# Bonus product in the full array, flag product with 128 columns, and another order of the attention cluster on TensorE

## The chip, the cores and the metric

The kernel runs on one core of a Trainium2 chip. The metric is the device time of one execution in microseconds; lower is better. A measurement of this kernel can tell a difference of about 0.2% (0.67 us) from no change.

## What is computed

The reference chains three blocks. The change touches the first, a recurrence over 768 steps for 2 batches and 8 heads of 48 channels:

```
for t in range(S):
    cur = einsum('bhd,bhe->bhde', u * k[t], v[t])
    y[t] = einsum('bhd,bhde->bhe', r[t], state + cur)
    state = w[t][:, :, :, None] * state + einsum('bhd,bhe->bhde', k[t], v[t])
```

Its output `y`, as a matrix of 2 x 768 tokens by 384 channels, goes through a gated feed-forward block (token shift, then `k = relu(xk @ w_k)`, `v = k*k @ w_v`, `sigmoid(xr @ w_r) * v`), and then through a second one (`h = gelu(x @ w_in)`, half of it normalised and mixed along the sequence by `w_sg`, gate, `x + gated @ w_out`).

## The kernel before

The 1536 tokens are cut into 12 units of 128 steps; two units make one of six stages (`T = 256` tokens). For each unit the recurrence is done in chunk form with small float32 products on TensorE. A tile holds two heads, each on 64 of the 128 partitions (48 used), so eight heads are four pairs (`PAIRS = 4`), and a pair's product is written as two products, one for each half of the partitions. The products of a unit `un` are:

- `scores(un)`: decayed keys times decayed receptance, 64 rows and 128 columns of weights for each head, into `ps`. VectorE then masks them into `att` (`mask`, a predicated copy of 128x1024).
- `keys_by_step(un)`: four transposes of the keys into `pkt`; ScalarE copies them into `k_tok` (`keys`).
- `bonus(un)`: `u` times (r*k), summed over a head's channels and spread over its 64 rows: 64x64 weights taken from `par`, which ScalarE's DMA queue loads at the start. The moving operand `rkp` is GpSimd's product r*k. The result goes to `pm` for units 0 and 1 and to `pkt` after that.
- `from_state(un)`: the state before the chunk, read by the receptance, 64x64 weights, into `py`. It is left out for units 0 and 6, where a batch begins.
- `add_state(un)`: what the chunk adds to the state, 128x64 weights, into `pu`. VectorE takes it on in `carry_on`. Left out for units 5 and 11.
- `from_chunk(un)`: masked scores times the values, 128x64 weights, added in `py` to what `from_state` left.
- `flag_of(s)`: the sum over partitions of a check on the decays, one column of weights (`ones`), into row 0 of `pu` beside the state's columns. ScalarE adds it up, and SyncE and VectorE branch on it; with these inputs the branch isn't taken.

Every float32 product of this kind runs as two passes, so the trace has 16 MATMUL records for the eight products of `bonus`. The large products (lines 297 to 299, called MLP here) are in another float32 format, use the full array (128 x 128 weights) and run as three products of one pass each.

The order on TensorE is written out by hand. After a head with warm-up products (line 293), the stage loop puts the attention products of later units between groups of MLP products. One cluster of it is `outputs(un)`, most often followed by `scores(un + 1)`:

```
def outputs(un):
    bonus(un)
    from_state(un)
    add_state(un)
    from_chunk(un)
```

All other engines have such hand-written orders as well, and semaphores tie them. Unit 1 is an exception (`MOVED = 1`): its cluster stands in the head as `from_state(1)`, `bonus(1)`, `from_chunk(1)`, `move_last(1)`.

Of the kernel before, what the change touches and what calls it, by code (L numbers as in the profile page):

```python
# [10 lines left out]
ACT = mybir.ActivationFunctionType  # L11
AX = mybir.AxisListType

P = 128
C = 128
SLOT = 64
# [5 lines left out]
N = 2  # L22
# [11 lines left out]
def build(nc, r, k, v, w, u, units, vT, params, w_k, w_v, w_r, w_in, wsgT, b_sg, w_out, outT):  # L34
# [18 lines left out]
    with ctx:  # L53
# [12 lines left out]
        def put(name, at, dims, dt=F32):  # L66
            at += -at % 8
            t = nc.alloc_sbuf_tensor_at(name, [P, *dims], dt, offset=base + 4 * at)
            n = 1
            for d in dims:  # L70
                n *= d
            return t, at + n
# [87 lines left out]
        assert e <= r3  # L160

        x2, e = put("x2", r3, [KT, B * S])
        par, e = put("par", e, [PAIRS * SLOT + 2 * KT + GT])
        u_b = par[:, 0:PAIRS * SLOT].rearrange("p (g e) -> p g e", g=PAIRS)
        mu = par[:, PAIRS * SLOT:PAIRS * SLOT + 2 * KT].rearrange("p (n t) -> p n t", n=2)
        gln = par[:, PAIRS * SLOT + 2 * KT:]
        omu, e = put("omu", e, [2, KT])
        outside, e = put("outside", e, [NU])
        flags, e = put("flags", e, [NU])
        flag, e = put("flag", e, [STAGES])  # L170
        ones, e = put("ones", e, [1])
        minus_one, e = put("minus_one", e, [1])
        half_neg, e = put("half_neg", e, [1])
        stats, e = put("stats", e, [ST, 6])
# [16 lines left out]
        def bonus_bank(un):  # L191

            return pm[un] if un < 2 else pkt
# [406 lines left out]
        def _(pe):  # L600
# [26 lines left out]
            def bonus(un):  # L627

                pe.wait_ge(s_par, 16)
                pe.wait_ge(rkp_done, un + 1)  # L630
                if un >= 2:
                    pe.wait_ge(ktok_done, states(un + 1))
                    pe.wait_ge(bonus_done, un)
                for g in range(PAIRS):
                    cols = slice(g * C, (g + 1) * C)
                    for h in range(2):
                        head = slice(h * SLOT, (h + 1) * SLOT)
                        mm = pe.matmul(bonus_bank(un)[head, cols], u_b[head, g], rkp[head, un % 2, cols],  # L638
                                       start=True, stop=True)
                mm.then_inc(c_mm, 1)  # L640

            def flag_of(s):

                pe.wait_ge(checked, N * (s + 1))
                pe.wait_ge(state_done, states(N * s + 1))
                pe.matmul(pu[0:1, STATE:STATE + N * (s + 1)], ones[:], outside[:, 0:N * (s + 1)],
                          start=True, stop=True).then_inc(flag_mm, 1)

            def add_state(un):
# [15 lines left out]
            def from_state(un):  # L665

                if place(un)[2] == 0:
                    return
                pe.wait_ge(state_done, states(un))
                if un >= 2:  # L670
                    pe.wait_ge(y_done, un)
                    pe.wait_ge(main_done, un)
                for g in range(PAIRS):
                    cols = slice(g * C, (g + 1) * C)
                    for h in range(2):
                        head = slice(h * SLOT, (h + 1) * SLOT)
                        pe.matmul(y_bank(un)[head, cols], state[head, (un - 1) % 2, g], r_in[head, un % 2, cols],  # L677
                                  start=g == 0, stop=False, skip_group_check=True)

            def from_chunk(un):  # L680

                first = place(un)[2] == 0
                pe.wait_ge(s_v[un % 3], 16 * (un // 3 + 1))
                pe.wait_ge(att_done, un + 1)
                if first and un >= 2:
                    pe.wait_ge(y_done, un)
                    pe.wait_ge(main_done, un)
                for g in range(PAIRS):
                    cols = slice(g * C, (g + 1) * C)
                    for h in range(2):  # L690
                        mm = pe.matmul(y_bank(un)[h * SLOT:(h + 1) * SLOT, cols], vb[:, un % 3, g, h, :],  # L691
                                       att[:, un % 2, h, cols], start=first and g == 0, stop=g == PAIRS - 1,
                                       skip_group_check=True)
                mm.then_inc(y_mm, 1)

            def move_last(un):

# [39 lines left out]

            def outputs(un):
                bonus(un)
                from_state(un)  # L740
                add_state(un)
                from_chunk(un)

            warm(pe, 4)
            scores(0)
# [105 lines left out]
        def _(act):  # L851
            act.dma_start(par[:], params).then_inc(s_par, 16)
            act.wait_ge(s_const, 7)
            act.activation(tables[:, 0:1], ones[:], ACT.Sigmoid).then_inc(s_sig, 1)

            def by_head(t):
                return t.rearrange("p (h e) -> p h e", h=2)
# [109 lines left out]
            for s in range(STAGES):  # L967
                a, b = 2 * s + 2, 2 * s + 3
                if s == 0:
                    gate(s, *RS[0])  # L970
                    high_weight(wv[0])
                    gate(s, *RS[1])
                    keys(1)
                    high_weight(wv[1])
                    key_high(s, 0)
                    check(a)
                    keys(a)
                    key_high(s, 1)
                    high_weight(wv[2])
                    check(b)  # L980
                    keys(b)
                    flag_out(s + 1)
                    key_high(s, 2)
                    high_weight(wv[3])
                    key_high(s, 3)
                    mix(s + 1)
                    keys(b + 1)
                elif s < STAGES - 1:
                    gate(s, *RS[0])
                    check(a)  # L990
                    check(b)
                    gate(s, *RS[1])
                    keys(b)
                    key_high(s, 0)
                    flag_out(s + 1)
                    for n in range(1, KG):
                        key_high(s, n)
                    mix(s + 1)
                    if b + 1 < NU:
                        keys(b + 1)  # L1000
                else:
                    gate(s, *RS[0])
                    gate(s, *RS[1])
                    act.activation(tables[:, 1:2], ones[:], ACT.Gelu_apprx_tanh).then_inc(s_sig, 1)
                    key_high(s, 0)
                    for n in range(1, KG):
                        high_weight(parts_of("win")[n - 1])
                        key_high(s, n)
                    split_x2(0)
# [331 lines left out]
def lay_out(inputs):  # L1341
# [5 lines left out]
    for un in range(B * S // C):  # L1347
# [13 lines left out]
                v_un[:, g, h, 0:D] = v[b, 2 * g + h, t]  # L1361
        units += [w_un, rkv_un.reshape(P, 3 * WIDE)]
        vT.append(v_un.reshape(C, WIDE))
    u_b = _np.zeros((P, PAIRS, SLOT), _np.float32)
    for g in range(PAIRS):
        for h in range(2):
            u_b[h * SLOT:h * SLOT + D, g] = u[2 * g + h][:, None]
    order = []
    for j in range(PAIRS - 1):
        for h in range(2):  # L1370
# [4 lines left out]
    arrays = {n: inputs[n] for n in "rkvwu"}  # L1375
    arrays["units"] = _np.concatenate(units, axis=1)
    arrays["vT"] = _np.concatenate(vT, axis=1)
    arrays["params"] = _np.concatenate([u_b.reshape(P, PAIRS * SLOT), *by_row], axis=1)
    arrays["moe_w_k"] = inputs["moe_w_k"][order]
    arrays["moe_w_v"] = inputs["moe_w_v"]  # L1380
    arrays["moe_w_r"] = inputs["moe_w_r"][order]
# [20 lines left out]
```

## Time and profile before

| | us |
|---|---|
| median of 3 runs (lowest, highest) | 333.68 (333.19, 333.71) |
| the profiled execution's own time | 332.61 |
| its span in the profile | 330.9 |
| TensorE matmul busy | 320.0 (97%) |
| TensorE weight load busy | 299.5 (91%) |
| VectorE busy | 197.2 (60%) |
| ScalarE busy | 151.0 (46%) |
| GpSimd busy | 98.1 (30%) |

The granted TensorE clock is full in all 40 slices of the page. Busy time of TensorE's matmuls counts overlapping records once. A matmul's record is longer than the distance to the next one (an MLP product's is 0.28 us long, and the next starts 0.12 us later), so costs on TensorE are read as distances between starts.

### The profile page before, as it was taken

What the parts mean: (1) busy time and instruction counts of PE and PEld (TensorE: products, weight loads), DVE (VectorE), ACT (ScalarE), POOL (GpSimd) and SP (SyncE); (2) the same over time, 40 slices, a digit from 0 to 9 for tenths busy, and PEclk for the clock granted to TensorE, in tenths of its full rate; (3) what the DMA queues carried; (4) which work ended last, traced back from release to release, by engine and by line L of the source; (5) the groups of instructions that cost most, each with busy time, mean ns of one, the idle gap of its engine ahead of it and who ended that gap; (6) DMA issues with size and microseconds to landing.
All of it is one profiled execution on the core that took longest, in us unless ns stands there. A gap on an engine that the chain in (4) does not pass through costs nothing.

```text
span 330.9 us, 6786 instructions
## 1 busy us (share of the span) xinstructions
PE 320.0 (97%) x2684; PEld 299.5 (91%) x2684; DVE 197.2 (60%) x331; ACT 151.0 (46%) x301; POOL 98.1 (30%) x94
## 2 busy tenths in 40 slices
PE   6987899999999999999999999999999999999996
PEld 2657889999999999999999998899999988999996
DVE  4869999983696398639416055991643546123432
ACT  5446844553845455465547592755113025311100
POOL 5530344004314211430032050672233018313220
PEclk9999999999999999999999999999999999999999
DMA  7979033232304401300006036000000210000012
GB/s 230 408 259 350 27 124 125 87 130 61 144 2 165 166 5 24 144 9 2 6 9 240 0 110 246 29 0 0 2 0 0 97 49 0 2 0 2 0 48 95
DMA packets 11153, 28.09 MB, mean 85 GB/s; under 512 B 1232, under 2 KB 5872, under 8 KB 9840
## 3 DMA queue, kind: packets, MB, share of 16 engines
q1 hardware_dynamic: 10976, 27.51, 23.7%
q8 instruction: 21, 0.34, 0.4%
q10 hardware_dynamic: 144, 0.14, 0.1%
q14 instruction: 12, 0.10, 0.1%
HBM read 24.74 MB, written 2.36 MB: 82 GB/s over the span
## 4 chain that ended last, share of the span: by engine, by line
PE 84%; DVE 7%; ACT 3%; issue 2%; DMA 2%; POOL 0%; SPq 0%; ACTq 0%; DVEq 0%
PE pm L297 16%; PE pm L298 15%; PE pm L299 15%; PE ps L613 3%; PE ps L297 3%; PE ps L299 3%; PE ps L298 3%; PE py L691 3%; PE pkt L638 3%; PE py L677 2%; PE pkt L297 2%; PE pkt L299 2%; PE pu L297 2%; PE pu L299 2%; PE pkt L298 2%
## 5 line engine op out<-in xcount | busy, mean ns | idle before, releaser
L542 POOL TENSOR_TENSOR k_l<-sq,k_h 128x512 fp32r<-128x512 f32 x24 | 31.9, 1332 | 79.2 <-ACT sq L944 79.2
L297 PE MATMUL pm<-xkr_h,wk_h 128*128 128x256 f32 x144 | 42.1, 292 | 0.0
L297 PE MATMUL pm<-k_h,wv_h 128*128 128x256 f32 x144 | 41.2, 286 | 0.4 <-POOL k_l L542 0.4
L299 PE MATMUL pm<-k_h,wv_l 128*128 128x256 f32 x144 | 40.7, 283 | 0.0
L298 PE MATMUL pm<-k_l,wv_h 128*128 128x256 f32 x144 | 40.7, 283 | 0.0
L298 PE MATMUL pm<-xkr_l,wk_h 128*128 128x256 f32 x144 | 40.7, 283 | 0.0
L299 PE MATMUL pm<-xkr_h,wk_l 128*128 128x256 f32 x144 | 40.7, 282 | 0.0
L533 POOL TENSOR_TENSOR rkp<-inw 128x512 f32<-128x512 f32 x12 | 15.3, 1281 | 62.7 <-DVE r_in L1132 62.7
L936 ACT ACTIVATE relu<-pm 128x512 f32<-128x512 f32 x24 | 14.3, 596 | 36.2 <-PE pm L299 36.1
L595 POOL TENSOR_TENSOR gated_l<-gf,gated_h 128x384 fp32r<-128x384 f32 x16 | 16.4, 1025 | 46.1 <-ACT gated_h L1055 36.1
L1187 DVE SCALAR_TENSOR_TENSOR xf<-X,omu,xf 128x256 f32<-128x256 f32 x36 | 19.5, 554 | 15.4 <-ACT xf L902 15.4
L297 PEld LDWEIGHTS pm<-xkr_h,wk_h 128*128 128x128 f32 x144 | 27.5, 191 | 1.0 <-issue 0.3
L297 PEld LDWEIGHTS pm<-k_h,wv_h 128*128 128x128 f32 x144 | 27.6, 192 | 0.7 <-issue 0.6
L1055 ACT CAST gated_h<-gf 128x384 fp32r<-128x384 f32 x16 | 8.2, 514 | 42.9 <-DVE gf L1330 42.9
L298 PEld LDWEIGHTS pm<-k_l,wv_h 128*128 128x128 f32 x144 | 27.6, 192 | 0.0
L299 PEld LDWEIGHTS pm<-k_h,wv_l 128*128 128x128 f32 x144 | 27.6, 192 | 0.0
L298 PEld LDWEIGHTS pm<-xkr_l,wk_h 128*128 128x128 f32 x144 | 27.6, 191 | 0.0
L299 PEld LDWEIGHTS pm<-xkr_h,wk_l 128*128 128x128 f32 x144 | 27.5, 191 | 0.0
L902 ACT ACTIVATE xf<-X,par 128x256 f32<-128x256 f32 x36 | 17.6, 503 | 5.9 <-DMA X<-y 5.9
L1139 DVE COPY_PREDICATED att<-upper,ps 128x1024 f32<-128x1024 uint32 x12 | 16.3, 1360 | 3.5 <-PE ps L613 3.4
L569 POOL TENSOR_TENSOR rstd<-vare,half_neg 128x1 f32<-128x1 f32 x12 | 9.3, 779 | 29.4 <-DVE vare L1308 29.4
L577 POOL TENSOR_TENSOR vn_l<-vf,vn_h 128x512 fp32r<-128x512 f32 x12 | 17.2, 1436 | 2.2 <-ACT vn_h L1016 2.2
(239 smaller groups left out, 880.4 us busy)
## 6 DMA issues: line engine op xcount, KB each, us to landing
inw<-in_units SPq DMA_DIRECT2D x10, 1026.5 KB, 5.0
vb<-in_vT SPq DMA_DIRECT2D x12, 256.0 KB, 5.0
wsg_raw<-in_wsgT SPq DMA_DIRECT2D x1, 2304.0 KB, 8.8
out_y<-y_out SPq DMA_DIRECT2D x12, 192.0 KB, 1.9
wk_raw<-in_moe_w_k SPq DMA_DIRECT2D x3, 512.0 KB, 9.9
wv_raw<-in_moe_w_v SPq DMA_DIRECT2D x4, 384.0 KB, 7.0
win_raw<-in_moe_w_in SPq DMA_DIRECT2D x3, 512.0 KB, 4.6
inw<-in_units SPq DMA_DIRECT2D x2, 512.0 KB, 5.5
```

Of the source, the lines that this page charges most:

```text
L297: pe.matmul(o, a_h, b_h, start=first and n == 0, stop=False, skip_group_check=True)
L298: pe.matmul(o, a_h, b_l, start=False, stop=False, skip_group_check=True)
L299: mm = pe.matmul(o, a_l, b_h, start=False, stop=last and n == len(pairs) - 1, skip_group_check=True)
L533: pool.tensor_tensor(rkp[:, un % 2], inw[:, un % 3, W1:W1 + WIDE], inw[:, un % 3, W1 + WIDE:W1 + 2 * WIDE], ALU.mult).then_inc(rkp_done, 1)
L542: pool.tensor_tensor(k2_l[:, 2 * n:2 * n + 2], sq[:, j % 2].rearrange("p (g t) -> p g t", g=2), k2_h[:, 2 * n:2 * n + 2], ALU.subtract).th ...
L577: pool.tensor_tensor(vn_l[:, t], vf[:, n % 2], vn_h[:, t], ALU.subtract).then_inc(vnl_done, 1)
L595: pool.tensor_tensor(gated_l[:, x, cols], gf[:, ng % 2], gated_h[:, x, cols], ALU.subtract).then_inc(gl_done, 1)
L613: mm = pe.matmul(ps[:, h, cols], k_in[head, p, cols], r_in[head, p, cols], start=True, stop=True)
L902: act.activation(xf[:, kt, n], X[:, s % 2, kt, 1:T + 1], ACT.Identity, scale=mu[:, n, kt:kt + 1]).then_inc(t_done, 1)
L936: act.activation(relu[:, j % 2], pm[bk][:], ACT.Relu).then_inc(m_free[bk], 1)
L1139: dve.copy_predicated(att[:, un % 2].rearrange("p h (g t) -> p h g t", g=PAIRS), upper[:].bitcast(U32).unsqueeze(1).unsqueeze(1).to_broadc ...
L1187: dve.scalar_tensor_tensor(out=xf[:, kt, n], in0=X[:, s % 2, kt, 0:T], scalar=omu[:, n, kt:kt + 1], in1=xf[:, kt, n], op0=ALU.mult, op1=AL ...
```

## The change

The weights of `bonus` become block-diagonal: `u_b` has 128 columns for each pair, with a head's `u` in its own 64x64 block and zeros elsewhere. One product in the full array then does both heads, so `bonus` issues four products where it issued eight. `par` grows from 266 to 522 columns, and so does the DMA that loads it. `flag_of` uses `ones` with 128 columns (a 128x128 memset on GpSimd where it was 128x1) and writes the sum into all 128 rows. In `outputs` the state reads move behind the chunk's product; so `from_chunk` now opens the accumulation in `py` and does the waiting for that bank, and `from_state` closes it and signals `y_mm`. For unit 1 the roles stay as they were.

```
-        par, e = put("par", e, [PAIRS * SLOT + 2 * KT + GT])
-        u_b = par[:, 0:PAIRS * SLOT].rearrange("p (g e) -> p g e", g=PAIRS)
+        par, e = put("par", e, [PAIRS * P + 2 * KT + GT])
+        u_b = par[:, 0:PAIRS * P].rearrange("p (g e) -> p g e", g=PAIRS)
...
-        ones, e = put("ones", e, [1])
+        ones, e = put("ones", e, [P])
...
                 for g in range(PAIRS):
                     cols = slice(g * C, (g + 1) * C)
-                    for h in range(2):
-                        head = slice(h * SLOT, (h + 1) * SLOT)
-                        mm = pe.matmul(bonus_bank(un)[head, cols], u_b[head, g], rkp[head, un % 2, cols],
-                                       start=True, stop=True)
+                    mm = pe.matmul(bonus_bank(un)[:, cols], u_b[:, g], rkp[:, un % 2, cols], start=True, stop=True)
                 mm.then_inc(c_mm, 1)
...
-                pe.matmul(pu[0:1, STATE:STATE + N * (s + 1)], ones[:], outside[:, 0:N * (s + 1)],
+                pe.matmul(pu[:, STATE:STATE + N * (s + 1)], ones[:], outside[:, 0:N * (s + 1)],
                           start=True, stop=True).then_inc(flag_mm, 1)
...
                 pe.wait_ge(state_done, states(un))
-                if un >= 2:
-                    pe.wait_ge(y_done, un)
-                    pe.wait_ge(main_done, un)
                 for g in range(PAIRS):
...
-                        pe.matmul(y_bank(un)[head, cols], state[head, (un - 1) % 2, g], r_in[head, un % 2, cols],
-                                  start=g == 0, stop=False, skip_group_check=True)
+                        mm = pe.matmul(y_bank(un)[head, cols], state[head, (un - 1) % 2, g], r_in[head, un % 2, cols],
+                                       start=un == MOVED and g == 0, stop=un != MOVED and g == PAIRS - 1,
+                                       skip_group_check=True)
+                if un != MOVED:
+                    mm.then_inc(y_mm, 1)
...
             def from_chunk(un):
 
-                first = place(un)[2] == 0
                 pe.wait_ge(s_v[un % 3], 16 * (un // 3 + 1))
                 pe.wait_ge(att_done, un + 1)
-                if first and un >= 2:
+                if un >= 2:
                     pe.wait_ge(y_done, un)
                     pe.wait_ge(main_done, un)
+                alone = place(un)[2] == 0 or un == MOVED
...
             def outputs(un):
                 bonus(un)
-                from_state(un)
                 add_state(un)
                 from_chunk(un)
+                from_state(un)
...
-    u_b = _np.zeros((P, PAIRS, SLOT), _np.float32)
+    u_b = _np.zeros((P, PAIRS, P), _np.float32)
     for g in range(PAIRS):
         for h in range(2):
-            u_b[h * SLOT:h * SLOT + D, g] = u[2 * g + h][:, None]
+            u_b[h * SLOT:h * SLOT + D, g, h * SLOT:(h + 1) * SLOT] = u[2 * g + h][:, None]
```

The order of TensorE's instructions at unit 2 in stage 0, behind the second group of key products of the MLP (`rkp,par` is `bonus`, `r_in,state` is `from_state`, `vb,k_tok` is `add_state`, `att,vb` is `from_chunk`; the shape is that of the output, x8 the number of products):

```order
-L638 MATMUL pkt<-rkp,par 64x128 x8
-L677 MATMUL py<-r_in,state 64x128 x8
-L661 MATMUL pu<-vb,k_tok 64x64 x8
-L691 MATMUL py<-att,vb 64x128 x8
+L636 MATMUL pkt<-rkp,par 128x128 x4
+L658 MATMUL pu<-vb,k_tok 64x64 x8
+L688 MATMUL py<-att,vb 64x128 x8
+L671 MATMUL py<-r_in,state 64x128 x8
 L613 MATMUL ps<-r_in,k_in 128x128 x8
 L624 MATMUL pkt<-ident,k_in 128x128 x4
```

The eight state reads stand last in the cluster now, behind the chunk's product and in front of the next unit's scores.

The head of TensorE's order, before, from the scores of unit 1 on (`outside,ones` is `flag_of`):

```order
L613 MATMUL ps<-r_in,k_in 128x128 x8
L638 MATMUL pm<-rkp,par 64x128 x8
L646 MATMUL pu<-outside,ones 1x2
L691 MATMUL pm<-att,vb 64x128 x8
L677 MATMUL py<-r_in,state 64x128 x8
L638 MATMUL pm<-rkp,par 64x128 x8
L691 MATMUL py<-att,vb 64x128 x8
```

And the same place of the change:

```order
L613 MATMUL ps<-r_in,k_in 128x128 x8
L636 MATMUL pm<-rkp,par 128x128 x4
L643 MATMUL pu<-outside,ones 128x2
L688 MATMUL pm<-att,vb 64x128 x8
L671 MATMUL py<-r_in,state 64x128 x8
L636 MATMUL pm<-rkp,par 128x128 x4
L688 MATMUL py<-att,vb 64x128 x8
```

Here nothing has moved; the two bonus products and the flag have changed their shapes. The orders of the other engines are the same but for the sizes of `par` and `ones`.

## Rows read from the trace of the kernel before

**Rows 1.** The page's busy times, share of the span and instructions
```profile
PE 320.0 (97%) x2684; PEld 299.5 (91%) x2684; DVE 197.2 (60%) x331; ACT 151.0 (46%) x301; POOL 98.1 (30%) x94
```

**Rows 2.** Stretches: length, busy of PE, PEld, DVE, ACT, POOL; clock, DMA, GB/s
```profile
42.00:202.00 160.00, 159.62 (x1669) 152.87 (x1666) 105.79 (x177) 88.93 (x186) 41.05 (x32) 1.00 0.26 89
202.00:331.00 129.00, 125.93 (x697) 121.36 (x695) 58.34 (x103) 37.06 (x66) 41.97 (x40) 1.00 0.08 25
```

**Rows 3.** Waits of TensorE from 42 us to the end: total us, times, longest
```profile
PE pm L297 <- POOL k_l L542: 0.4, 1, 0.4
```

**Rows 4.** Timeline of TensorE around the cluster of unit 3: start us, length us
```profile
46.16 0.28 PE L299 MATMUL pm<-xkr_h,wk_l 128*128 128x256 f32 x1
46.37 1.09 PE L638 MATMUL pkt<-rkp,par 64*64 64x128 f32 x16
47.30 1.04 PE L677 MATMUL py<-r_in,state 64*64 64x128 f32 x16
48.27 0.69 PE L661 MATMUL pu<-vb,k_tok 128*64 128x64 f32 x16
48.78 1.04 PE L691 MATMUL py<-att,vb 128*64 128x128 f32 x16
49.76 0.39 PE L297 MATMUL pm<-xkr_h,wk_h 128*128 128x256 f32 x1
49.98 0.28 PE L298 MATMUL pm<-xkr_l,wk_h 128*128 128x256 f32 x1
```

**Rows 5.** The same timeline around the cluster of unit 2
```profile
37.97 1.09 PE L638 MATMUL pkt<-rkp,par 64*64 64x128 f32 x16 [0.18 <-issue]
...
39.86 0.69 PE L661 MATMUL pu<-vb,k_tok 128*64 128x64 f32 x16
41.20 1.10 PE L691 MATMUL py<-att,vb 128*64 128x128 f32 x16 [0.65 <-DVE att L1139]
42.22 1.16 PE L613 MATMUL ps<-r_in,k_in 64*128 64x128 f32 x16
```

**Rows 6.** Timeline of VectorE: the mask of unit 2
```profile
39.69 1.36 DVE L1139 COPY_PREDICATED att<-upper,ps 128x1024 f32<-128x1024 uint32 x1
```

**Rows 7.** Timeline of weight loads: six float32 passes in the full array
```profile
20.44 0.74 PEld L701 LDWEIGHTS py<-y,moves 128*128 128x128 f32 x6 [0.70 <-issue]
21.11 0.30 PEld L293 LDWEIGHTS pm<-one,ident 128*128 128x128 f32 x2
```

**Rows 8.** Timeline of TensorE around the flag of stage 2
```profile
72.30 0.28 PE L299 MATMUL pm<-xkr_h,wk_l 128*128 128x256 f32 x1
72.51 0.19 PE L646 MATMUL pu<-outside,ones 128*1 128x6 f32 x2
...
72.86 0.28 PE L298 MATMUL pm<-xkr_l,wk_h 128*128 128x256 f32 x1
```

**Rows 9.** Timeline of TensorE in the head
```profile
15.97 1.09 PE L691 MATMUL pm<-att,vb 128*64 128x128 f32 x16
17.00 1.09 PE L677 MATMUL py<-r_in,state 64*64 64x128 f32 x16
```

**Rows 10.** DMA queues from 1.8 to 4.4 us, and the page's row on par
```profile
q1 hardware_dynamic: 222, 0.58, 75.0%
q10 hardware_dynamic: 144, 0.14, 16.4%
...
par<-in_params ACTq DMA_DIRECT2D x1, 133.0 KB, 3.5
```

**Rows 11.** Timelines of VectorE and ScalarE in the head
```profile
0.79 0.41 ACTq L852 DMA_DIRECT2D par<-in_params  x1
...
4.26 1.23 DVE L1110 TENSOR_TENSOR_SCAN prod<-inw,one 128x516 f32<-128x516 f32 x1 [4.26 <-DMA inw<-in_units]
...
21.41 0.56 DVE L1176 TENSOR_TENSOR X<-py,inw 128x384 f32<-128x384 f32 x1
...
22.24 0.91 ACT L902 ACTIVATE xf<-X,par 128x256 f32<-128x256 f32 x2 [4.14 <-DMA X<-y]
```

More of the change, by code:

```diff
@@ L162, in build @@
         x2, e = put("x2", r3, [KT, B * S])
-        par, e = put("par", e, [PAIRS * SLOT + 2 * KT + GT])
-        u_b = par[:, 0:PAIRS * SLOT].rearrange("p (g e) -> p g e", g=PAIRS)
-        mu = par[:, PAIRS * SLOT:PAIRS * SLOT + 2 * KT].rearrange("p (n t) -> p n t", n=2)
-        gln = par[:, PAIRS * SLOT + 2 * KT:]
+        par, e = put("par", e, [PAIRS * P + 2 * KT + GT])
+        u_b = par[:, 0:PAIRS * P].rearrange("p (g e) -> p g e", g=PAIRS)
+        mu = par[:, PAIRS * P:PAIRS * P + 2 * KT].rearrange("p (n t) -> p n t", n=2)
+        gln = par[:, PAIRS * P + 2 * KT:]
         omu, e = put("omu", e, [2, KT])
@@ L691, in from_chunk @@
                         mm = pe.matmul(y_bank(un)[h * SLOT:(h + 1) * SLOT, cols], vb[:, un % 3, g, h, :],
-                                       att[:, un % 2, h, cols], start=first and g == 0, stop=g == PAIRS - 1,
-                                       skip_group_check=True)
-                mm.then_inc(y_mm, 1)
+                                       att[:, un % 2, h, cols], start=un != MOVED and g == 0,
+                                       stop=alone and g == PAIRS - 1, skip_group_check=True)
+                if alone:
+                    mm.then_inc(y_mm, 1)
             def move_last(un):
@@ L853, in _ @@
             act.wait_ge(s_const, 7)
-            act.activation(tables[:, 0:1], ones[:], ACT.Sigmoid).then_inc(s_sig, 1)
+            act.activation(tables[:, 0:1], ones[:, 0:1], ACT.Sigmoid).then_inc(s_sig, 1)
             def by_head(t):
@@ L1003, in _ @@
                     gate(s, *RS[1])
-                    act.activation(tables[:, 1:2], ones[:], ACT.Gelu_apprx_tanh).then_inc(s_sig, 1)
+                    act.activation(tables[:, 1:2], ones[:, 0:1], ACT.Gelu_apprx_tanh).then_inc(s_sig, 1)
                     key_high(s, 0)
@@ L1377, in lay_out @@
     arrays["vT"] = _np.concatenate(vT, axis=1)
-    arrays["params"] = _np.concatenate([u_b.reshape(P, PAIRS * SLOT), *by_row], axis=1)
+    arrays["params"] = _np.concatenate([u_b.reshape(P, PAIRS * P), *by_row], axis=1)
     arrays["moe_w_k"] = inputs["moe_w_k"][order]
```

## Prediction

> **What bounds the kernel now.** I read the page's busy times first. TensorE is busy for 97% of the span, and no other engine for more than 60% [rows 1]. Such a share is an average, so I looked at stretches next. From 42 to 202 us TensorE is busy 159.62 us of 160, and from 202 us on 125.93 of 129, of which the last piece is the tail of the output [rows 2]. The view of waits confirms it: from 42 us to the end TensorE waits once, for 0.4 us [rows 3]. The reader should see that from 42 us on TensorE's own time is the kernel's time. Each 0.1 us added to its instructions there, or taken from them, arrives at the end.
>
> Before 42 us it is otherwise. The first work starts when a DMA has landed, at 4.26 us on VectorE [rows 11], and unit 2's `from_chunk` waits 0.65 us for the mask `att`, which VectorE finishes at 39.69 + 1.36 = 41.05 us [rows 5, 6]. So TensorE is tied to VectorE once more at 41.05 us, and only what moves that point, or comes behind it, counts.
>
> **The change part by part.** The sum is made against the profiled execution's own 332.61 us. The median of the runs, 333.68, lies 1.07 above it; I add the change to the median.
>
> *What a change of array shape costs.* The records name the part of the array: 64*64, 128*64, 128*128. Where it changes, the pairs of starts are further apart. `from_chunk` of unit 3 takes 48.78 to 49.76 = 0.98 with a change behind it and none ahead; that of unit 0 takes 15.97 to 17.00 = 1.03 with one on both sides [rows 4, 9]. So coming in costs 0.05. `bonus` of unit 3 takes 0.93 with a change ahead and none behind, so sixteen passes take 0.88, and going out costs 0.10. MLP products follow each other by 0.12; going out of them takes 0.21 (46.16 to 46.37), and coming back 0.22 (49.76 to 49.98), so 0.09 and 0.10 more [rows 4].
>
> *Bonus in the full array.* Eight passes in place of sixteen, which looks like half. But the sixteen run two by two: 0.88 us for eight pairs is 0.11 for a pair. A full-array float32 pass with 128 moving columns has a row too, the products with `moves`: six passes from 20.44 to 21.11, 0.112 each [rows 7]. Eight take 0.89. The two halves already ran side by side, so nothing is gained in the product itself.
>
> The Trainium skill ("TensorE: Matmul & The Clock Gate", Back-to-back issue gap) gives about 81 ns for a product with 128 moving columns in a sustained stream. By it the eight passes would take 0.65 us, and the sum would be about 2.2 us lower over the nine clusters behind unit 2's. The trace disagrees, with 0.112 us for a pass of this very kind.
>
> *The cluster of unit 3.* Before: 0.21 + 0.93 + 0.97 + 0.51 + 0.98 + 0.22 = 3.82 [rows 4]. After: MLP to bonus has no change of shape, 0.12. Bonus with a change behind it, 0.89 + 0.10 = 0.99. `add_state`, 0.51, as before with a change ahead. `from_chunk` 0.98. `from_state`, now with a change on both sides, 0.05 + 0.88 + 0.10 = 1.03. MLP 0.22. Sum 3.85, so 0.03 more. The change of shape that the bonus no longer needs ahead of it comes back between the chunk's product and the state reads: three changes before, three after. With scores behind the cluster both have one more. Eight clusters are like this one (units 3, 4, 5 and 7 to 11; without `add_state` the difference is the same), +0.24. Unit 6 has no state reads, so there the saved change isn't given back: 0.09 + 0.05 + 0.88 + 0.10 - 0.99 = 0.13 less. Together +0.11. No row shows a change from 64*64 to 128*128 or 64*128; if it cost nothing, the eight would save 0.10 each more (-0.8), and if it cost as much again, +0.8. All other kinds in the rows agree within 0.01 us, so I take 0.10.
>
> *The flag.* It takes 72.30 to 72.86 = 0.56 where two steps of 0.12 would be 0.24, so 0.32 for a product of a few columns: two changes of shape [rows 8]. In the full array it needs none, and is two passes of at most 0.112: 0.22. Five flags stand behind 42 us: 5 x (0.32 - 0.22) = -0.50. Bounds: -0.3 (some of it stays) to -1.0 (passes with so few columns cost 0.02).
>
> *The cluster of unit 2.* This is where the new order costs. Before, TensorE ran the state reads while the mask was being made, and then waited 0.65 us. Now they stand behind `from_chunk`, which can't start before `att` (41.05 us) however early TensorE gets there. Bonus and additions end by 37.97 + 0.99 + 0.51 = 39.5, and the wait grows from 0.65 to about 1.7 us. From 41.20 on the chunk's product takes 1.02 as before [rows 5], and then 1.03 of state reads come before the scores that stood at 42.22. Queued behind them are the scores of unit 3, the mask of unit 3 and all MLP products. Nothing hides this: TensorE has no wait behind 42 us that could shrink but the one of 0.4, which comes from a chain that is moved with it. So +1.03, between 0.9 and 1.1. At no other unit does the mask bind: unit 3's chunk starts without a wait at 48.78 [rows 4], and moves up by one block only.
>
> *The larger par.* It has 256 more columns, 131 KB. Its 144 packets run between 1.8 and 4.4 us beside those that VectorE's first scan waits for, with 91% of the 16 engines' time taken; its own share is 16.4% of 2.6 us, 0.43 us [rows 10]. It is nearly doubled, so the scan's data land up to 0.42 us later if all of the new bytes are served ahead of them, and 0 if none. Both land within 0.2 us of each other (0.79 + 3.5 = 4.3 for par, 4.26 for the scan's start [rows 10, 11]), so they are served side by side. I take +0.35. From the scan the chain runs through VectorE without a pause, so this moves 41.05 and all that follows.
>
> The Trainium skill ("DMA: Bandwidth & Descriptors", the queue model) says that each DMA engine goes round the queues that have work, packet by packet. By that rule most of par's new bytes come ahead of the scan's last ones, which is the upper end; the trace, with both landing together, agrees.
>
> *The rest of the head.* Bonus 0, the flag and unit 0's chunk stay within 0.05: 0.89 + 0.22 against 1.02 + 0.12. Unit 1's bonus gets changes ahead and behind, some 0.15 later; its `X` is written at 21.41 + 0.56 = 21.97, with 0.27 to spare to 22.24 [rows 11]. I take +0.05 for both. The wider memset of `ones` (0.1 us or so) is over long before 4.26 us.
>
> Sum: 0.11 - 0.50 + 1.03 + 0.35 + 0.05 = +1.04. That gives 333.65 for a profiled execution, and 333.68 + 1.04 = 334.7 for the median, 0.3% slower.
>
> **The rivals.**
> 1. *The head hides par.* The extra bytes fall into gaps of the DMA engines (9% are free). Then the sum is +0.7: 334.4. For it: the share isn't 100%. Against it: the two transfers land together. Chance 0.15.
> 2. *The stall of unit 2 isn't new time*, because the mask comes earlier than in the old trace or TensorE arrives there later anyway. Then the sum is about 0: 333.7. Against it: VectorE is at work without a pause up to the mask, and its order is unchanged. Chance 0.08.
> 3. *Faster: a change in one direction only (rows or columns) costs less than one in both.* In the new order each change inside a cluster is in one direction. If both changes that the state reads now have were free, eight clusters would save 0.3 each, -2.4: 332.3. It decides from 0.22 us per cluster on, where the sum falls under -0.67. Against it: 64*64 to 128*64 (rows only) costs 0.10 in unit 3, and 128*64 to 128*128 (columns only) 0.10 as well, no less than the others [rows 4]. Chance 0.05.
> 4. *Faster: a full-array pass is paced by its moving columns.* An MLP product has 256 and takes 0.12 [rows 4]; half of that is 0.06, eight passes 0.48, and nine clusters would save 0.41 each: -3.7, 331.0. Against it: the six passes at 0.112 [rows 7]. Chance 0.02. (The Trainium skill's 81 ns, in the section named above, would stand between the two.)
> 5. *Slower still: a change that no row shows (64*64 straight to 128*128 or 64*128) is dearer.* With 0.1 us more in each of nine clusters, 335.6. Chance 0.1.
>
> The forecast keeps 0.6, with 334.2 to 335.2 as its own range.
>
> **How the numbers follow.** A measurement can tell about 0.2%, 0.67 us: 333.0 to 334.35 is no change. Slower holds the forecast but for a sliver (0.57), half of rival 1 and all of rival 5: 0.74. Same: that sliver, half of rival 1 and rival 2: 0.19. Faster: rivals 3 and 4, 0.07. The range leaves out rivals 3 and 4, most of 5 and some of 2: 333.7 to 335.4.
>
> **What would show it.** In the new profile: `from_chunk` of unit 2 waits about 1.7 us for `att`; its scores start 1.0 us later than the mask's shift alone explains; bonus blocks take 0.99 from start to start and follow MLP by 0.12; the cluster of unit 3 takes 3.85; a flag takes 0.22 over its neighbours; the first scan starts near 4.6 us. The prediction is wrong if the scan starts at 4.26 as before, if unit 2's wait stays under 1 us, or if the cluster of unit 3 is shorter than 3.7.

## The result and the profile after

The changed kernel takes 334.07 us (median of 22 runs, 333.72 to 334.43), the kernel before 333.33 (22 runs, 332.44 to 333.90). The ratio is 1.0022 with a 95% interval of 1.0015 to 1.0029: slower by 0.74 us, inside the predicted range of 333.7 to 335.4 and on the predicted side, less than the 1.04 us of the sum. It isn't a clear hit: 334.07 lies under the forecast's own range (334.2 to 335.2) and, counted from the older median 333.68, inside the band 333.0 to 334.35 that the prediction calls no change, to which it gave 0.19. The median of before over 22 runs is 0.35 lower than that of the first three. The profiled execution took 333.90, 1.29 above that of before.

The page of the changed kernel: the span, the busy times, and ScalarE's DMA queue, which carries `par`:

```profile
span 332.2 us, 6594 instructions
...
PE 320.1 (96%) x2588; PEld 300.8 (91%) x2588; DVE 198.7 (60%) x331; ACT 151.0 (45%) x301; POOL 97.8 (29%) x94
...
q10 hardware_dynamic: 144, 0.27, 0.2%
```

TensorE has 96 records fewer (48 products of two passes) and is busy as long as before [rows 1]: half as many bonus passes take the same time. The queue carries 0.13 MB more.

The timeline of TensorE at unit 2, where [rows 5] are the rows of before:

```profile
38.72 1.13 PE L636 MATMUL pkt<-rkp,par 128*128 128x128 f32 x8 [0.27 <-issue]
39.78 0.69 PE L658 MATMUL pu<-vb,k_tok 128*64 128x64 f32 x16
41.82 1.09 PE L688 MATMUL py<-att,vb 128*64 128x128 f32 x16 [1.35 <-issue]
42.84 1.09 PE L671 MATMUL py<-r_in,state 64*64 64x128 f32 x16
43.87 1.16 PE L613 MATMUL ps<-r_in,k_in 64*128 64x128 f32 x16
```

VectorE's mask for that unit:

```profile
40.37 1.35 DVE L1137 COPY_PREDICATED att<-upper,ps 128x1024 f32<-128x1024 uint32 x1
```

The chunk's product now idles 1.35 us and starts 0.10 after the mask's end at 41.72. The prediction's 1.7 is counted between starts; counted so it is 1.52 (39.78 + 0.52 to 41.82). The profile puts that wait down to "issue", but the mask is what ends just ahead of it, as in [rows 5, 6]. The mask starts 0.68 later than in [rows 6]; unit 3's scores start 1.65 later than in [rows 5] (43.87 for 42.22). So 0.97 us are new at this place.

The cluster of unit 3, to be held against [rows 4]:

```profile
47.71 0.28 PE L299 MATMUL pm<-xkr_h,wk_l 128*128 128x256 f32 x1
47.83 1.05 PE L636 MATMUL pkt<-rkp,par 128*128 128x128 f32 x8
48.81 0.69 PE L658 MATMUL pu<-vb,k_tok 128*64 128x64 f32 x16
49.33 1.04 PE L688 MATMUL py<-att,vb 128*64 128x128 f32 x16
50.30 1.09 PE L671 MATMUL py<-r_in,state 64*64 64x128 f32 x16
51.32 0.39 PE L297 MATMUL pm<-xkr_h,wk_h 128*128 128x256 f32 x1
51.55 0.28 PE L298 MATMUL pm<-xkr_l,wk_h 128*128 128x256 f32 x1
```

From start to start: 0.12 into the bonus, 0.98 for it, 0.52, 0.97, 1.02, 0.23: 3.84 us in all, against 3.82 before.

The flag of stage 2, for [rows 8]:

```profile
73.90 0.28 PE L299 MATMUL pm<-xkr_h,wk_l 128*128 128x256 f32 x1
74.02 0.28 PE L643 MATMUL pu<-outside,ones 128*128 128x6 f32 x2
...
74.36 0.28 PE L298 MATMUL pm<-xkr_l,wk_h 128*128 128x256 f32 x1
```

0.46 us where it was 0.56. And the head, for [rows 11]: VectorE's first scan and the two rows on which ScalarE's first product with `mu` hangs:

```profile
4.76 1.23 DVE L1108 TENSOR_TENSOR_SCAN prod<-inw,one 128x516 f32<-128x516 f32 x1 [4.76 <-DMA inw<-in_units]
...
22.19 0.56 DVE L1174 TENSOR_TENSOR X<-py,inw 128x384 f32<-128x384 f32 x1
...
22.92 0.91 ACT L900 ACTIVATE xf<-X,par 128x256 f32<-128x256 f32 x2 [4.46 <-DVE X L1174]
```

The scan starts 0.50 later. ScalarE's product starts 0.68 later and is released by `X` of unit 1, no longer by the DMA as in [rows 11]. `X` itself is 0.78 late (22.19 for 21.41), 0.28 of it behind the scan. That comes from TensorE, at unit 1's bonus and chunk, before:

```profile
17.92 1.04 PE L638 MATMUL pm<-rkp,par 64*64 64x128 f32 x16
18.89 1.09 PE L691 MATMUL py<-att,vb 128*64 128x128 f32 x16
```

and now:

```profile
18.58 1.16 PE L636 MATMUL pm<-rkp,par 128*128 128x128 f32 x8
19.67 1.09 PE L688 MATMUL py<-att,vb 128*64 128x128 f32 x16
```

The full-array bonus takes 1.09 from start to start for 0.97, and the state reads ahead of it 1.02 for 0.92 (17.56 to 18.58, before 17.00 to 17.92). Unit 0's bonus, flag and chunk add 0.07 (0.99 + 0.22 for 1.02 + 0.12). Of these 0.28 us 0.10 are hidden: the product starts 0.17 after the end of `X` (22.19 + 0.56 = 22.75, 22.92), so before, `X` had 0.10 to spare and not 0.27.

The whole way of these 1.3 us in the two traces: +0.50 at the first scan, +0.18 in the rest of the head, +0.97 at unit 2, and -0.35 from unit 3's scores to the end (332.2 - 43.87 = 288.33 for 330.9 - 42.22 = 288.68). The medians differ by 0.74 only. The experiments are about that gap as much as about the terms.

### The profile page after: what moved, and what is told of

It is laid out like the page before. It is cut to its first block, busy times and chain, and to the rows that moved or that the text cites. A ratio compares the mean times of both kernels' runs of the same rounds, so it can differ in the third digit from the quotient of the medians.

```text
span 332.2 us, 6594 instructions
## 1 busy us (share of the span) xinstructions
PE 320.1 (96%) x2588; PEld 300.8 (91%) x2588; DVE 198.7 (60%) x331; ACT 151.0 (45%) x301; POOL 97.8 (29%) x94
## 4 chain that ended last, share of the span: by engine, by line
PE 88%; DVE 5%; ACT 3%; issue 2%; DMA 1%; POOL 0%; ACTq 0%; DVEq 0%
PE pm L297 16%; PE pm L298 16%; PE pm L299 16%; PE ps L613 4%; PE ps L297 3%; PE ps L298 3%; PE ps L299 3%; PE py L688 3%; PE py L671 3%; PE pkt L636 3%; PE pu L658 2%; PE pkt L297 2%; PE pkt L298 2%; PE pkt L299 2%; PE pu L297 2%
```

## The experiments

Each kernel was timed in 6 or 12 runs beside the kernel before on the same chip. Every run also lists the mean clock granted over the span, which turned out to matter. For reading them together, this table has five figures of each profile (us): the start of the first scan, the start of the mask of unit 2, the start of the scores of unit 3, the span, and the rest from those scores to the end of the span, in which TensorE alone sets the time.

| kernel | first scan | mask of unit 2 | scores of unit 3 | span | rest | median of runs |
|---|---|---|---|---|---|---|
| before | 4.26 | 39.69 | 42.22 | 330.9 | 288.68 | 333.33 |
| changed | 4.76 | 40.37 | 43.87 | 332.2 | 288.33 | 334.07 |
| par wide only | 4.74 | 40.05 | 43.20 | 331.9 | 288.70 | 333.64 |
| order only | 4.06 | 39.64 | 43.15 | 333.1 | 289.95 | 334.98 |
| unit 2 in old order | 4.68 | 40.28 | 43.60 | 331.9 | 288.30 | 333.84 |
| all in old order | 4.99 | 40.57 | 43.08 | 331.4 | 288.32 | 333.67 |
| before, 4 products filled in | 4.15 | 39.50 | 42.39 | 331.1 | 288.71 | 333.25 |
| changed, 4 filled in | 4.61 | 40.23 | 43.72 | 332.0 | 288.28 | 334.00 |
| flag wide, 4 filled in | 4.30 | 40.38 | 43.27 | 331.5 | 288.23 | 332.73 |
| unit 2 old, 4 filled in | 4.83 | 40.47 | 43.55 | 331.9 | 288.35 | 333.61 |
| before, 2 filled in | 4.29 | 39.61 | 42.13 | 330.8 | 288.67 | 332.76 |
| changed, 2 filled in | 4.70 | 40.30 | 43.79 | 332.1 | 288.31 | 333.99 |
| unit 2 old, 2 filled in | 4.84 | 40.45 | 42.97 | 331.3 | 288.33 | 332.96 |
| flag wide, par late, 2 filled in | 3.75 | 40.59 | 43.12 | 331.3 | 288.18 | 332.59 |

**Par alone.** The kernel before with `par` padded by zeros to the new width:

```
-    arrays["params"] = _np.concatenate([u_b.reshape(P, PAIRS * SLOT), *by_row], axis=1)
+    arrays["params"] = _np.concatenate([u_b.reshape(P, PAIRS * SLOT), _np.zeros((P, PAIRS * SLOT), _np.float32), *by_row], axis=1)
```

> The kernel before, with par widened from 266 to 522 columns by zeros that nothing reads; all else as before. If par's new bytes come ahead of the data of the first scan, the scan starts near 4.7 us in the profile where it was 4.26, and the time rises by 0.4 to 0.5 us. If they fall into free time of the DMA engines, both stay and the time is that of before within 0.2 us.

Measured: the scan starts at 4.74 for 4.26, so the DMA term is real, and somewhat above its upper bound of 0.42. One pair of profiles would not carry that, but all of them do: the scan starts at 4.06 to 4.30 in the five with the small par loaded first (4.21 on the average), and at 4.61 to 4.99 in the eight with the large one (4.77). The time is 333.64 against 333.35 of the kernel before beside it, ratio 1.0011 (0.9998 to 1.0024): some 0.3 us, which the interval doesn't tell from none. The trace held something unlooked for. A stretch of this profile (length, busy of PE, PEld, DVE, ACT and POOL with counts, granted clock, DMA share, GB/s):

```profile
31.00:34.00 3.00, 2.71 (x24) 2.59 (x25) 2.93 (x5) 0.97 (x2) 0.25 (x1) 0.59 0.85 340
```

In the profile of before it reads:

```profile
31.00:34.00 3.00, 3.00 (x36) 2.80 (x37) 2.93 (x5) 0.61 (x2) 0.61 (x1) 1.00 0.65 230
```

and its timeline has these rows of TensorE behind the wait for `k_tok`:

```profile
30.93 0.69 PE L661 MATMUL pu<-vb,k_tok 128*64 128x64 f32 x16 [2.12 <-ACT k_tok L888]
...
33.89 1.16 PE L613 MATMUL ps<-r_in,k_in 64*128 64x128 f32 x16
```

The timeline of TensorE with par wide, behind the transposes of unit 1 and then at unit 2:

```profile
31.29 0.95 PE L661 MATMUL pu<-vb,k_tok 128*64 128x64 f32 x16 [2.13 <-ACT k_tok L888]
...
32.55 0.41 PE L298 MATMUL pm<-xkr_l,wk_h 128*128 128x256 f32 x1
32.77 0.41 PE L299 MATMUL pm<-xkr_h,wk_l 128*128 128x256 f32 x1
...
35.73 1.16 PE L613 MATMUL ps<-r_in,k_in 64*128 64x128 f32 x16
...
42.22 1.05 PE L691 MATMUL py<-att,vb 128*64 128x128 f32 x16
43.20 1.16 PE L613 MATMUL ps<-r_in,k_in 64*128 64x128 f32 x16
```

TensorE waits 2.13 us for `k_tok`. When it goes on, its clock is at half, the lower of its two levels, 1.2 GHz: products of 0.41 us that follow each other by 0.21 where they were 0.28 and 0.12. The scores behind that group of key products start at 35.73 for 33.89: 1.84 us later, 0.36 of which were there at the end of the wait (31.29 for 30.93), so the drop costs 1.5. At unit 2 TensorE therefore comes later than the mask (41.40) and doesn't wait for it: the chunk's product starts 0.82 behind the mask's end, where 0.15 is usual, so 0.67 of the 1.5 us get through. In the profile of before the same wait of 2.12 us was not followed by a drop. So two kinds of executions exist, and the mean clock tells them apart: in the profiles it is 0.995 where the drop occurred (three) and 0.999 or 1.000 where not; that it is the same drop in the executions that were only timed is inferred from this. Of the 99 timed executions of the kernel before whose clock is listed (29, 35 and 35, on three chips), 71 had a mean of 0.994 or 0.995 and took 333.54 (median), 28 had 0.999 or 1.000 and took 332.51. (The expectation below that speaks of 18 of 26 miscounts: it was 21 of 29.) Of the changed kernel 11 had it (334.15) and 11 not (333.99).

By kinds, par alone costs 0.86 us where there was no drop (7 runs, 333.31; before 8 runs, 332.45) and 0.17 with it (333.79 for 333.62). Also, the 1.0 us between the two kinds of the kernel before is more than the 0.67 that the trace shows of the drop. The kinds differ in the head as well: in the three profiles with the drop unit 0's scores start without a wait behind TensorE's warm-up products, in the three without it and without the filling described below they wait 0.20 to 0.60 us for VectorE. What ties the two together is not shown.

So TensorE's lateness and its wait at unit 2 are alternatives. Where the clock has dropped, the time that the new order loses at unit 2 had been lost before TensorE got there.

**Order alone.** The new order with the 64x64 bonus, the flag of one column and the small par:

```
-                    mm = pe.matmul(bonus_bank(un)[:, cols], u_b[:, g], rkp[:, un % 2, cols], start=True, stop=True)
+                    for h in range(2):
+                        head = slice(h * SLOT, (h + 1) * SLOT)
+                        mm = pe.matmul(bonus_bank(un)[head, cols], u_b[head, g], rkp[head, un % 2, cols],
+                                       start=True, stop=True)
```

> The new order of the cluster with the old products (bonus 64x64, flag with one column, small par). If changes of array shape are what counts, each cluster now has four of them where it had three: unit 3 takes 3.82 + 0.15 = 3.97 us, eight clusters add 1.2 us, unit 2 adds 1.0 for its wait, in all about +2.2 us. If the order costs only by the wait of unit 2, +1.0 us. If shapes that differ in one direction only changed cheaply, less than +1.0.

Measured: 334.98 (6 runs), ratio 1.0064 (1.0045 to 1.0083), so 1.6 us over before where 2.2 was expected. The cluster of unit 3:

```profile
47.28 1.09 PE L638 MATMUL pkt<-rkp,par 64*64 64x128 f32 x16
48.30 0.69 PE L661 MATMUL pu<-vb,k_tok 128*64 128x64 f32 x16
...
49.79 1.09 PE L674 MATMUL py<-r_in,state 64*64 64x128 f32 x16
50.81 0.39 PE L297 MATMUL pm<-xkr_h,wk_h 128*128 128x256 f32 x1
```

The bonus takes 1.02 and the state reads 1.02, where 0.93 and 0.97 stand in [rows 4]: each is now shut in between two changes of shape. The rest behind unit 3's scores is 1.27 us longer than before; 1.2 was expected for eight clusters. The order by itself saves nothing. It adds a change of shape to each cluster, and the wide bonus takes one away. Unit 2's loss hardly shows, since five of the six runs had the drop: their median is 335.01, 1.39 over the 21 runs of before beside them that had it too (333.62), little more than those 1.27.

**Unit 2 alone in the old order.**

```
+        STATE_FIRST = (MOVED, 2)
...
             def outputs(un):
                 bonus(un)
+                if un in STATE_FIRST:
+                    from_state(un)
                 add_state(un)
                 from_chunk(un)
-                from_state(un)
+                if un not in STATE_FIRST:
+                    from_state(un)
```

(with the start and stop flags, the wait for the bank and the signal moved accordingly)

> The changed kernel, but in unit 2's cluster alone the state reads stand ahead of the additions and the chunk's product again. If the longer wait of unit 2 for its mask is new time, this is 1.0 us faster than the changed kernel (333.1 where that is 334.07). If the wait is made good later, both are the same.

Measured: 333.84, 0.2 under the changed kernel and not 1.0. A miss, if one looks at medians. By the clock it is a hit, if on few runs: the 4 runs without the drop have a median of 332.96, the changed kernel's 11 such runs 333.99, so 1.03 us; the 8 with the drop 333.95, against 334.15, so 0.20.

**All clusters in the old order**, with the wide products (`STATE_FIRST = tuple(range(NU))`).

> The changed kernel's wide bonus, flag and par with the old order in all clusters. By the count of changes of shape, three for the cluster of unit 3 in this order too, it takes 3.85 us as in the changed kernel, and the time equals that of the kernel whose unit 2 alone has the old order, within 0.2 us (1.0 us under the changed kernel). If the order is worth something by itself (changes in one direction only are cheaper), it is slower than that one by 0.1 us or more per cluster, 0.8 us in all.

Measured: 333.67, ratio to before 1.0019 (1.0006 to 1.0032), 0.17 from the kernel with unit 2 alone in the old order, with 332.99 and 333.89 by the clock. The rest is 288.32 for 288.30 there and 288.33 in the changed kernel. Which way round the products stand doesn't matter behind unit 2; what counts is the number of changes of shape, and it is the same. The rival of cheap changes in one direction is out.

**Filling the wait.** If idleness precedes the drop, work in its place should keep the clock up, and show the change at its full price. Four warm-up products went into the wait for `k_tok` at unit 1, in four kernels:

```
                     keys_by_step(1)
+                    warm(pe, 4)
                     add_state(1)
```

> The kernel before, with four warm-up products (line 293, 1.7 us at full clock, results not used) in the 2.1 us in which TensorE waits for k_tok at unit 1. In 18 of 26 timed executions of the kernel before the mean clock was 0.995, and in the profiles with that mean the granted clock was at 0.5 from about 31.4 to 34.8 us; those executions took 1.0 us longer. If what precedes the drop is the idle stretch, no execution has it now, and all are near 332.5. If the drop has nothing to do with it, two in three still have it and the median stays near 333.4.

Measured: 333.25, ratio to before 1.0005 (0.9993 to 1.0017). All 12 runs have a mean clock of 1.000 or 0.999, so the drop is gone, yet the time isn't near 332.5. The timeline shows my error:

```profile
28.43 3.60 PE L293 MATMUL pm<-one,ident 128*128 128x512 f32 x8
31.96 0.69 PE L661 MATMUL pu<-vb,k_tok 128*64 128x64 f32 x16
```

Four products are eight passes, 3.5 us, not the 1.7 that the expectation says. They overfill the wait: the additions start 1.0 us later (31.96 for 30.93), and [rows 5] show that TensorE had 0.8 left at unit 2 (39.86 + 0.52 to 41.20). That explains some 0.2 to 0.4 us. The profiled execution, 332.77, was the fastest of the twelve; what the others took on top, up to 333.76, no trace shows, but the head, which differs between executions as told below, could be the place.

> The changed kernel with the same four products in the same wait. At full clock it took 333.99, with the drop 334.15, as TensorE has 1.4 us to spare ahead of unit 2's mask. If the drop is gone, 334.0, and the distance to the kernel before with the same filling is the full price of the change, 1.5 us, twice what was measured without the filling. The rival, that the change costs 0.7 us whatever the clock does, gives 0.7 us over it.

Measured: 334.00, ratio 1.0026 (1.0015 to 1.0038). The time is as expected; the distance to the filled kernel before is 0.75 and not 1.5, since that one was itself late.

> The changed kernel with unit 2 in the old order and with the filling. If the state reads behind unit 2's mask cost 1.0 us at full clock and less only where the clock had dropped, this is 1.0 us faster than the changed kernel with the filling (333.0). Without filling the difference of the medians was 0.2 us.

Measured: 333.61, 0.39 under the changed kernel with the same filling, again because TensorE comes late by the filling.

The fourth, the kernel before with the wide flag alone:

```
-                pe.matmul(pu[0:1, STATE:STATE + N * (s + 1)], ones[:], outside[:, 0:N * (s + 1)],
+                pe.matmul(pu[:, STATE:STATE + N * (s + 1)], ones[:], outside[:, 0:N * (s + 1)],
```

> The kernel before with the filling, and the flag product alone widened to 128 columns. By the prediction's term the five flags behind 42 us save 0.5 us against the filled kernel before (332.0 where that is 332.5). If the passes are paced by their weight loads more slowly than the rows of before suggest, or nothing of a change of shape is saved, 0.0 to 0.2.

Measured: 332.73, 0.52 under the filled kernel before; the rest is 288.23 for 288.71. This doesn't hang on unit 2, so the term of the flag stands. In this kernel the wide flag costs something in the head: between unit 0's bonus (64*64) and chunk (128*64) it takes 0.32 (16.43 to 16.75) where the narrow one took 0.12.

**Filling it with two products** (1.7 us) gives the test that the four had spoilt.

> The kernel before with two warm-up products in the wait for k_tok where the earlier filling had four: four took 3.5 us (line 293 runs as two passes of 0.43 us), 1.1 us more than the wait, and so cost what they were to save. Two take 1.7 us and fit. If the drop of the clock follows the idle stretch, it is gone here too, and the median is 332.5, as in the executions of the kernel before without a drop, 0.9 under its median. If 0.6 us of idleness is enough, the drop stays in part and the median is near 333.3.

Measured: 332.76 (332.41 to 333.84), 0.53 under before by the medians; the ratio is 0.9993, and its interval, 0.9981 to 1.0006, doesn't exclude that nothing was gained. No run has the drop. The wait is filled but for 0.41 us, and TensorE waits for the mask of unit 2 again:

```profile
31.00:34.00 3.00, 3.00 (x36) 2.80 (x36) 2.93 (x5) 0.61 (x2) 0.69 (x1) 1.00 0.92 343
```

```profile
28.55 1.88 PE L293 MATMUL pm<-one,ident 128*128 128x512 f32 x4
30.85 0.69 PE L661 MATMUL pu<-vb,k_tok 128*64 128x64 f32 x16 [0.41 <-ACT k_tok L889]
...
41.11 1.09 PE L691 MATMUL py<-att,vb 128*64 128x128 f32 x16 [0.55 <-DVE att L1140]
42.13 1.16 PE L613 MATMUL ps<-r_in,k_in 64*128 64x128 f32 x16
```

> The changed kernel with two products in the wait. TensorE waits for unit 2's mask at either clock, so the filling gives nothing: 334.0, 1.5 us over the filled kernel before. If the change costs 0.7 us whatever the clock does, it is 0.7 over that.

Measured: 333.99, ratio to before 1.0027 (1.0015 to 1.0039), and 1.23 us above the filled kernel before. The filling gives the changed kernel nothing, and before 0.5. That is the price of the change with the clock held up, well over the 0.74 of the plain medians. It is not quite the 1.5 expected, which is also the distance between the runs without a drop when nothing is filled (333.99 for 332.51, 1.48); the two profiles with filling are 1.3 apart in span, as are the two without. So the price is 1.2 to 1.5, and the sum's 1.04 lies under all of these.

> The changed kernel with unit 2 in the old order and two products in the wait. By the price of the state reads at full clock 1.0 us under the changed kernel with the same filling, 333.0. If the reads behind the mask cost only what the medians without filling showed, 0.2 us under it.

Measured: 332.96 (332.79 to 333.30), 1.03 under the changed kernel with the same filling. At unit 2 the changed kernel with two products has these rows,

```profile
41.75 1.09 PE L688 MATMUL py<-att,vb 128*64 128x128 f32 x16 [1.33 <-issue]
...
43.79 1.16 PE L613 MATMUL ps<-r_in,k_in 64*128 64x128 f32 x16
```

and with unit 2 in the old order these:

```profile
39.78 1.09 PE L675 MATMUL py<-r_in,state 64*64 64x128 f32 x16
...
41.94 1.09 PE L692 MATMUL py<-att,vb 128*64 128x128 f32 x16 [0.46 <-DVE att L1145]
42.97 1.16 PE L614 MATMUL ps<-r_in,k_in 64*128 64x128 f32 x16
```

The same state reads lie ahead of the mask's end there, and the scores start at 42.97.

**A better version.** The kernel before with the wide flag, two products in the wait, and `par` loaded behind the first unit's decays:

```
-            act.dma_start(par[:], params).then_inc(s_par, 16)
...
+            act.wait_ge(s_in[0], 16)
+            act.dma_start(par[:], params).then_inc(s_par, 16)
             check(0)
```

> The candidate for the best version: the kernel before (its order, its 64x64 bonus, its small par) with the flag product in 128 columns, par loaded only after the first unit's decays have landed, and two products in the wait. The flag gives 0.5 us. Out of the way of the first load, par gives up to 0.4 us: the first scan starts near 3.9 us. In all 331.7 to 332.0, 1.3 to 1.7 under the median of before. If par was never in the way, 332.0; if its late landing holds up the bonus of unit 0, over 332.5.

Measured: 332.59 (331.66 to 333.08), ratio to before 0.9980 (0.9969 to 0.9992), the best of all kernels here and 1.5 us under the changed one. But it is only 0.17 under the kernel before with two products, where 0.8 was hoped for. The flag gave its part (rest 288.18 for 288.67) and took 0.20 back in the head, as above (16.67 to 16.99). The scan starts 0.5 earlier (3.75 for 4.29), and nothing of that arrives: the mask of unit 2 stands at 40.59, later than in any other profile (this profiled execution, 333.05, was the second slowest of the twelve). The late `par` isn't the reason: unit 0's bonus follows its scores without a wait. Its head:

```profile
2.98 6.58 PE L293 MATMUL pm<-one,ident 128*128 128x512 f32 x8 [2.98 <-POOL upper L522]
9.49 1.16 PE L613 MATMUL ps<-r_in,k_in 64*128 64x128 f32 x16
```

And the same two rows of the profile of before:

```profile
2.88 5.34 PE L293 MATMUL pm<-one,ident 128*128 128x512 f32 x8 [2.88 <-POOL upper L522]
8.45 1.16 PE L613 MATMUL ps<-r_in,k_in 64*128 64x128 f32 x16 [0.23 <-DVE r_in L1132]
```

The eight warm-up passes ahead of unit 0's scores first follow each other by 0.85 us and later by 0.43, and when the pace doubles differs between executions: their weight loads are 0.85 apart up to 5.60 in the profile of before, and up to 8.27 here. That looks like the clock's two levels, but the granted clock is given as 1.00 in these stretches, so it is not shown. The passes last to 9.5 here, to 8.2 in the profile of before. When they end late, TensorE and not the scan sets the head. So a shift of the scan arrives in full only in executions in which they end early. The wide `ones` adds to it: its memset, 0.20 us for 0.10, puts the first warm-up product at 2.98 for 2.88.

## Why the prediction was right, point by point

*What bounds the kernel.* Right. Behind unit 3's scores every profile follows from TensorE's instructions alone: the rest is 288.67 to 288.71 with the old products and order, 288.18 and 288.23 with the wide flag alone, 288.28 to 288.35 with the wide bonus and flag in either order, 289.95 with the order alone. Bonus and order together thus cost about 0.1, where 0.11 was predicted (the span is given to 0.1 us).

*Changes of shape and the bonus.* Right to some 0.01 us: 0.98 for the bonus (0.99 predicted), 3.84 for the cluster (3.85), the state reads 1.02 (1.03). The pairs of 64x64 passes had run side by side, so half the passes save nothing. With -0.35 behind unit 3's scores for the -0.39 of the sum, rivals 3, 4 and 5 fall as well.

*The flag.* Right: 0.46 from start to start for 0.46 (0.56 - 0.10), and 0.5 us for the five.

*Unit 2.* The mechanism is right and shown by undoing it. The size, +1.03, holds in executions without the clock's drop (0.97 in the traces, 1.03 between medians, with and without filling) and is 0.20 in those with it, seven in ten of before and one in two of the changed kernel. The sentence of the prediction that fell short is that TensorE can't start the chunk's product before the mask "however early TensorE gets there": true, but it often gets there late. The trace of one execution could not show that, but one number ahead of the prediction hinted at it: the profiled execution lay 1.07 us under the median. The prediction added the change to the median and took that distance for a plain offset; by the later runs it is the distance between the two kinds of executions (333.54 and 332.51). Rival 2 had the idea, that "TensorE arrives there later anyway", with a chance of 0.08; it is the better part of why 0.74 was measured where the traces show 1.3.

*The larger par.* Mechanism right: +0.48 with par alone, 0.50 in the changed kernel, more than the 0.35 taken and more even than its bound of 0.42 (which came from the packets' mean time). What arrives of it at the end differs: about 0.3 with par alone and an interval that reaches to zero, which mixes 0.86 without the drop and 0.17 with it. The reason given for its arriving is wrong. From the scan on VectorE doesn't run "without a pause"; in the trace of before it waits for TensorE in the head:

```profile
14.94 1.37 DVE L1139 COPY_PREDICATED att<-upper,ps 128x1024 f32<-128x1024 uint32 x1 [1.04 <-PE ps L613]
...
19.01 0.69 DVE L1149 TENSOR_TENSOR inw<-pm,inw 128x512 f32<-128x512 f32 x1 [1.14 <-PE pm L638]
```

So the head hangs on TensorE too, and where its warm-up products end late they set it. Rival 1 (the head hides par, 0.15) has its reason refuted, since the scan does start later, but its outcome comes about in such executions.

*The rest of the head.* Too small: 0.18 for 0.05. Unit 1's bonus and what stands around it came 0.21 later and not 0.15, unit 0's part 0.07 and not nothing (coming from the scores' shape its bonus takes 0.99 and not 0.89), and `X` had 0.10 to spare and not 0.27, as the sum left out the 0.17 us between its end and ScalarE's start.

*The sum.* From the traces: +0.50 + 0.18 + 0.97 - 0.35 = +1.30; predicted 0.35 + 0.05 + 1.03 - 0.39 = 1.04. With the clock held up the medians differ by 1.23. The terms of the head were too small by 0.28. In the plain medians it is 0.74, because the drop makes most executions of before late already. So that 1.04 came near the measured 0.74 is in part luck: a sum too small by 0.3 met an effect that was not in it and took off 0.5 to 0.7.

Open: how much of the 0.5 us of `par` arrives on the average, since no run held the pace of the first warm-up products fixed; why the drop follows the same wait in some executions and not in others; and where the 0.3 us come from by which the two kinds of executions differ beyond the drop.

## What to carry to other kernels

A product of two halves that already run side by side in their own parts of the array isn't sped up by merging them; count the weight loads and passes in time, and then the changes of array shape, each of which costs here 0.15 to 0.2 us whichever direction it goes. Before moving work behind a wait, ask what it had been covering: the state reads cost nothing as long as they stood ahead of the mask, and 1.0 us behind it, in executions in which TensorE got there in time. And where two executions of one kernel differ by more than the effect, look at the granted clock of each stretch before the medians are compared; filling an idle stretch of TensorE with products that are thrown away took the drop out of every run here, and 0.5 us off the median, though the interval of that gain reaches to zero.

## What the runs showed of the hardware that was not expected

- After the same 2.1 us of idleness (and a wait of 0.7 to 0.9 us that ended some 4 us ahead of it), the granted clock was at half from about 31.5 us (0.59 on the average of 31 to 34) to 34.9 in one profile, and by the mean clock so in 71 of 99 timed executions of the kernel before, and not in the others. With 0.4 us of idleness left, it dropped in none of 12, nor in any of 36 with the same filling in other kernels, nor in any of the 48 with four products.
- The drop costs 1.5 us of TensorE's time (1.84 less 0.36, as above). Of that 0.67 gets past unit 2's mask in the trace with the old order; between the two kinds of executions the medians differ by 1.0 in the kernel before and by 0.2 in the changed one.
- 131 KB more on ScalarE's DMA queue put the landing of a transfer on SyncE's queue off by 0.48 us in one pair of profiles and by 0.56 on the average of all. Worked out from [rows 10], their own share of the 16 engines' time is an estimated 0.42.
